# Identity turns ahead of the first decays, and turns of r and k moved behind the output products

## The reference

```python
def _attn_ref(r, k, v, w, u):          # 4 batches, 8 heads, 768 steps, head size 48
    for t in range(S):
        cur = einsum('bhd,bhe->bhde', u * kt, vt)
        y[:, :, t] = einsum('bhd,bhde->bhe', rt, state + cur)
        state = wt[..., None] * state + einsum('bhd,bhe->bhde', kt, vt)

def _moe_ref(x, w_in, w_out):          # 3072 tokens, 384 -> 2048 -> 384
    h = x @ w_in
    return np.maximum(0.01 * h, h) @ w_out

def _moe2_ref(x, expert_emb, tau, w1, w2):   # 8 experts, 384 -> 1024 -> 384
    expert_idx = argmax(normalised(x) @ normalised(expert_emb).T / tau)
    out[token] = gate * (relu(x @ w1[e]) @ w2[e])     # e: the token's expert
```

## Time and profile before

| | |
|---|---|
| median of 3 runs | 822.52 us (821.8 to 823.58) |
| profiled execution: its time | 823.92 us |
| profiled execution: its span | 822.2 us |
| TensorE busy | 808.1 us, 98% of the span |
| weight loads | 758.6 us, 92% |
| VectorE, ScalarE, GpSimd busy | 566.1, 437.7 and 204.3 us |
| mean granted TensorE clock | 0.998 |

### The profile page before, as it was taken

One profiled execution on the slowest core, in us unless ns is written; L12 is line 12 of the kernel. 1 busy time (PEld: TensorE's weight loads), 2 busy tenths in 40 slices (PEclk: granted clock), 3 DMA queues, 4 the chain that ended last, 5 costly groups with the idle time before them and its releaser, 6 DMA issues.

```text
span 822.2 us, 18213 instructions
## 1 busy us (share of the span) xinstructions
PE 808.1 (98%) x5573; PEld 758.6 (92%) x5573; DVE 566.1 (69%) x1329; ACT 437.7 (53%) x923; POOL 204.3 (25%) x288
## 2 busy tenths in 40 slices
PE   7999999999999999999999999999999999999996
PEld 6899999999999999999999999999989888998896
DVE  6899787789889889989979855735541512455462
ACT  5776464464375375465465344653643633565463
POOL 5621111122003003103112002303542422434423
PEclk9999999999999999999999999999999999999999
DMA  9975431347334243243330012215432413386391
GB/s 210 212 181 100 76 74 27 58 91 89 65 74 55 48 85 54 39 95 47 50 73 14 1 43 88 98 39 182 143 102 79 156 44 123 108 276 204 95 309 60
DMA packets 199868, 81.52 MB, mean 99 GB/s; under 512 B 170047, under 2 KB 187814, under 8 KB 199651
## 3 DMA queue, kind: packets, MB, share of 16 engines
q1 hardware_dynamic: 173826, 66.98, 34.1%
q0 software_dynamic: 4544, 10.85, 4.1%
q10 hardware_dynamic: 21408, 2.61, 2.4%
HBM read 115.85 MB, written 11.63 MB: 155 GB/s over the span
## 4 chain that ended last, share of the span: by engine, by line
PE 90%; issue 3%; ACT 2%; DVE 2%; DMA 1%; POOL 1%; SPq 0%; POOLq 0%; DVEq 0%; ACTq 0%
PE bank L1133 24%; PE bank L1112 23%; PE bank L1185 13%; PE bank L1226 12%; PE bank L1038 3%; PE bank L1066 3%; PE bank L1202 3%; PE bank L1059 2%; PE bank L990 2%; PE bank L1046 1%; PE bank L1167 1%; PE bank L1075 1%; DMA stage<-in_moe_w_dram 1%; DMA Rn<-in_r_dram 1%; PE bank L1158 0%
## 5 line engine op out<-in xcount | busy, mean ns | idle before, releaser
L1112 PE MATMUL bank<-xhl,WRh 128*128 128x384 f32 x768 | 219.0, 339 | 0.2 <-issue 0.2
L1112 PEld LDWEIGHTS bank<-xhl,WRh 128*128 128x128 f32 x768 | 141.3, 188 | 0.6 <-issue 0.6
L1133 PE MATMUL bank<-WRh,gh 128*128 128x384 f32 x384 | 135.8, 354 | 0.0
L1112 PE MATMUL bank<-xhl,WRl 128*128 128x384 f32 x384 | 130.0, 339 | 0.0
L1133 PE MATMUL bank<-WRh,gl 128*128 128x384 f32 x384 | 129.8, 338 | 0.0
L1133 PE MATMUL bank<-WRl,gh 128*128 128x384 f32 x384 | 129.7, 338 | 0.0
L1528 ACT CAST gh<-gw 128x384 fp32r<-128x384 f32 x128 | 65.3, 510 | 103.4 <-DVE gw L1870 85.7
L1522 ACT COPY gw<-bank 128x384 f32<-128x384 f32 x128 | 61.3, 479 | 108.7 <-PE bank L1112 108.4
L1877 DVE TENSOR_TENSOR gl<-gw,gh 128x384 fp32r<-128x384 f32 x128 | 72.1, 563 | 59.2 <-ACT gh L1528 56.7
L2045 DVE TENSOR_TENSOR hl<-bank,hh 128x512 fp32r<-128x512 f32 x56 | 36.2, 686 | 85.4 <-ACT hh L1563 85.0
L1870 DVE SCALAR_TENSOR_TENSOR gw<-gw 128x384 f32<-128x384 f32 x128 | 72.9, 569 | 19.1 <-ACT gw L1522 19.0
(11 more groups left out here) (202 smaller groups left out, 1633.6 us busy)
## 6 DMA issues: line engine op xcount, KB each, us to landing
stage<-in_moe_w_dram SPq DMA_DIRECT2D x96, 768.0 KB
Kn<-in_k_dram SPq DMA_DIRECT2D x24, 192.0 KB, 3.7
Vn<-in_v_dram SPq DMA_DIRECT2D x24, 192.0 KB, 3.5
x_moe<-x2s SPq DMA_DIRECT2D x24, 192.0 KB, 3.0
Rn<-in_r_dram SPq DMA_DIRECT2D x21, 192.0 KB, 2.8
wraw<-in_moe_w_out_dram SPq DMA_DIRECT2D x4, 768.0 KB, 7.2
eraw<-in_moe_w_dram SPq DMA_DIRECT2D x4, 768.0 KB, 7.6
Wn<-in_w_dram SPq DMA_DIRECT2D x152, 16.0 KB
```

What stands on the lines that cost most here:

```text
L1112: mm = pe.matmul(bank[F_BANK[n % 2]][:, 0:GN], win(t_)[:, f // 4, k_, cols], xhl[G % 2][:, a, k_, :], start=(k_ == 0 and n_ == 0), stop=(k ...
L1133: mm = pe.matmul(bank[O_BANK[i]][:, 0:DM], a[:, z, cols], wout(t_)[:, f, :], start=(f == 0 and n_ == 0), stop=(f == FT - 1 and n_ == 2))
```

## The change

`warm(8, ...)` now stands in front of `turn_w(0)` and `warm(4, ...)` in front of `turn_w(1)`. Both write the bank of chunk 2's r, EARLY[2][1]. In the loop, the turns of r and k of chunks 4 to 8 now stand behind `out_part(n - LAG)` of the slot, where they stood between `feature(n)` and it; the turn of k of the chunks from 9 on stays where it was.

```diff
             def turn_rk(m):
 
-                if m < R_BLOCKED:
-                    turn_r(m)
+                turn_r(m)
                 turn_k(m)
...
                         for m in at(turn_at, n):
-                            turn_rk(m)
+                            if m >= R_BLOCKED:
+                                turn_k(m)
                         for m in at(score_at, n):
                             scores(m)
...
                     if n >= lo + LAG or (not first and n >= LAG):
                         out_part(n - LAG)
+                    if not first:
+                        for m in at(turn_at, n):
+                            if m < R_BLOCKED:
+                                turn_rk(m)
...
+            warm(8, EARLY[2][1])
             turn_w(0)
             pe.wait_ge(s_const, 4)
             turn_rk(0)
+            warm(4, EARLY[2][1])
             turn_w(1)
             turn_rk(1)
             scores(0)
```

## The result

The changed kernel takes 820.37 us, the median of 8 runs (820.06 to 821.26), the kernel before 822.86 us in the same comparison (8 runs, 821.8 to 823.92). The ratio is 0.9970 with a 95% interval of 0.9959 to 0.9981: 2.5 us less, 1.6 to 3.4 us by the interval. The forecast was 820.1 us, or 2.4 us less than the median shown then. The median alone does not tell the forecast from the rival in which only the moved turns pay: the 1.83 us of that rival lie within the interval too.

The account below looks back on a forecast made before the run. TensorE was taken as the bound nearly everywhere, with gains only in what it loses before about 115 us. From the median, 822.52 - 0.6 (warm turns) - 1.83 (moved turns) = 820.1 us; range 819.0 to 821.9 us.

Parts of the forecast that it names:

- the rival in which only the moved turns pay: Start: the clock's rise does not move, only slots 4 and 20 gain 1.83 us, giving 820.7 us; chance 0.22.
- The warm turns, 0.6 us of a possible 1.2: Start: twelve added turns raise TensorE's clock earlier, so mask(1) follows mask(0); 1.2 us, of which 0.6 credited.
- the cap by ScalarE: Start: ScalarE's copy at 19.03 us idles only 1.06 us for TensorE, the lower figure for the warm turns' gain.
- the gap of mask(1): Start: mask(1) could start at 16.09 in place of 17.42 us, a gain of 1.33 us.
- The half credit: Start: the median run may already rise early, so 0.6 of 1.2 us was taken; ends 0 and 1.33.
- The rule that spoke against it: Start: turns do not count for the clock gate as matmuls do, making the warm turns' term 0.
- The cover of the warm turns: Start: added turns end 0.2 us before w is turned, so cost nothing; with no cover, 2.6 us.
- The moved turns, 1.83 us: Slots 4 and 20: output products put ahead cover stalls of 1.00 and 0.83 us in full.
- The spare time at scores(4): Loop: TensorE reaches scores(4) at 54.5 us, Kt(4) is done at 54.20 us, leaving 0.3 us to spare.
- the rival in which only the warm turns pay: Loop: VectorE paces slots 5 to 20, the 1.83 us return as waits, giving 821.9 us; chance 0.15 including nothing.
- the slower rival: Loop: late turns stop VectorE, up to 1.57 us in each of five slots, 7.9 us; chance 0.07.
- the cover of 1.7 us: Slot 9: moved pair would end at 71.55 us, VectorE takes it at 73.28; about 1.4 us with the drain.

Follow-up runs that it names:

- four executions of before: The unedited kernel before, profiled as shown and three more times: 823.92, 823.55, 822.12 and 822.70 us.
- the one with products there: Changed kernel with its first eight warm turns replaced by six products of a tile of ones with itself: 820.61 us, ratio 0.9972 to the kernel before.
- the fourth execution of before: The kernel before, no edit, third further profile: 822.70 us.
- the second execution of the changed kernel: The changed kernel, no edit, profiled once more: 821.13 us.
- three repeats of before: The kernel before, no edit, profiled three further times: 823.55, 822.12 and 822.70 us.
- without the 18 turns: Changed kernel without the 18 warm turns ahead of chunk 2's r, which the kernel before has too: 821.86 us, ratio 0.9982 to the kernel before.

## Why the prediction was right

**The warm turns, 0.6 us of a possible 1.2.** The mechanism held. With a rise by about 8.3 us scores(1) waited for Kt(1), mask(1) moved up behind mask(0), and the start is 1.26 us shorter, between the ends 1.06 and 1.33 that the cap by ScalarE and the gap of mask(1) gave. The half credit was an inference from one profile lying 1.40 us above the median; the repeats bear it out, as two of four executions of before had no late rise, and in these nothing was left to gain (33.27 and 33.34 against 33.23 us). Over the four, scores(3) start at 33.86 us on average, 0.64 us behind the mean of the changed kernel's two. That this lies so near 0.6 is in part luck, with four executions of two kinds; by medians the size isn't shown (1.2 us with the warm turns alone, in an interval that touches none; 0.5 us between the ratios of the changed kernel and of the moved turns alone). The warm turns don't make the best start faster. What they may do is to make the good case the usual one: the six profiles with warm turns ahead of chunk 0's w and the one with products there all rose by 8.3 us, of six without them three did by 8.6 us and three did not. If the warm turns changed nothing, all three late ones would fall among those six in one case of 14, so this is likely and not proven.

**The rule that spoke against it.** In the changed kernel every product that TensorE runs before the rise is a turn, and it rose between 8.09 and 8.32 us; in the fourth execution of before twelve turns and two idle stretches were enough. Turns do bring the clock up here. The rule of the Trainium skill, page "TensorE: Matmul & The Clock Gate", section on PE-mode transpose, that turns do not count for the gate as matmuls do, is contradicted by these rows for float32 turns. The rival in which only the moved turns pay loses that ground. Its other form, that the rise comes when it comes whatever is put ahead of it, is what the one case in 14 leaves.

**The cover of the warm turns** was put at 0.2 us and is 0.39 us, since the eight turns load in 1.57 us and not in 1.74. Sixteen turns showed the price beyond it: the start is 1.16 us longer where w is turned 1.3 us later.

**The moved turns, 1.83 us.** Measured between landmarks it is 1.76 us with them alone and 1.75 us in the profile of after; by the ratio of the moved turns alone it is 2.0 us. Slot 4 gave 1.00 us to the hundredth or two in six profiles of seven. The spare time at scores(4) was read as 0.3 us, and that was too much. In the profile of after Kt(4) is complete at 52.95 us and scores(4) start at 53.19 us:

```profile
51.67 0.68 DVE L1823 TENSOR_TENSOR Rh<-bank,Fi 128x512 f32<-128x512 f32 x1
52.27 0.68 DVE L1829 TENSOR_TENSOR Kt<-bank,Xi 128x512 f32<-128x512 f32 x1
```

```profile
53.19 0.97 PEld L1037 LDWEIGHTS bank<-Rh,Kt 64*128 64x128 f32 x16 [0.25 <-issue]
```

That is 0.24 us. But where scores do wait for `Kt`, they start 0.11 us behind its end (14.81 and 14.92 us in chunk 1 of the same profile, 53.38 and 53.49 us in the second execution), so only 0.13 us of it is spare. The sum took the end of `Kt` and the start of the scores with nothing between. In the second execution of the changed kernel VectorE was 0.43 us late, the spare time was used up, and 0.2 us came back as a wait: the mechanism of the rival in which only the warm turns pay, at a fifth of its price of 1.0 us.

VectorE's lateness for r and k, the slower rival, did not appear: behind its first wait, for chunk 0's w, none of VectorE's waits in the profile of after is for a turn. In slot 9 the moved pair ends at 69.36 us and VectorE takes it at 71.04 us, the cover of 1.7 us that was read from the earlier trace rows. No run moved the turns further, so how much of that cover is real isn't measured.

**The sum.** Against the profiled execution I had 820.9 us and the profile of after took 820.14. 3.03 us of it are the terms, forecast 3.03, since 1.26 us against 1.2 and 1.75 against 1.83 make up for each other. The rest of the span's gain, 0.9 us, arose after 761 us, in two places. From the turns at 761.28 us to those of the last tile at 808.28 us it takes 47.00 us, against 46.58 in the profile of after: TensorE waited 0.8 us for `xgl` in the profile of before and not in that of after. From the turns of the last tile to the end of the span it takes 13.9 us, against 13.5. Both vary between executions of one kernel: the second profile of the changed kernel waits 0.7 us for `xgl` again and has 47.06 and 13.7 us, and three repeats of before wait 0.6 to 0.9 us and have 46.15 to 47.24 and 13.5 to 13.6 us. So they are no part of the change. What sets them wasn't tested.

## What to carry to other kernels

A start that TensorE shares with a slower partner is bounded by that partner: count how many of the microseconds that a faster clock saves are used before TensorE waits for it (here 1.3 of 2.2), and how thick the cover of the added work is, since what goes beyond it comes out behind it. Before a term is built on one profile's clock, look at how the profiled time stands to the median, and profile the kernel before more than once: a rise late by chance is paid back only in the executions that had it. A stall for another engine's copy goes if independent products of the same slot, here 1.57 us of them, can be put ahead of the waiting instruction. What uses the delayed result must have spare time for the delay, and from a spare time read between two rows the few tenths that a start always needs behind its release go off (here 0.11 us of 0.24).

## What the runs showed of the hardware

- The moment of TensorE's rise differs between executions of one program by more than 5 us: by 7.3, by 8.6, past 10.8 and past 12.6 us for the kernel before, while the loads that wait for chunk 1's w and r start within 0.4 us of each other. With warm work ahead of chunk 0's w it lay between 5.3 and 8.3 us in seven profiles.
- TensorE's turns against a float32 identity bring the clock up: in the changed kernel nothing but turns ran before the rise at 8.1 to 8.3 us. They also keep it up: without the 18 turns, an idle of 2.81 us and 1.7 us of work at full pace behind it, the same 16 products took 1.57 us in place of 0.85, at a granted clock of 0.50.
- Six float32 products of 128x128 by 128 columns are listed as 12 weight loads of 218 ns each at the low level, two for each product, where a turn of the same size has one.
- The granted clock read 1.00 in the stretches before the rise, while the same work took twice the time; only the durations show this first low level, though the fall without the 18 turns is in the column, as 0.50. Windows of the profile of before, TensorE alone (stretch, length, busy, granted clock, DMA share, GB/s):

```profile
4.00:6.80 2.80, 2.79 (x12) 1.00 0.97 202
...
7.40:12.50 5.10, 4.93 (x28) 1.00 1.16 237
```
